# Keys times values in quarter tiles, and another order at the seam of two loops, in a three-stage sequence model kernel

## What is computed

```python
batch, n_heads, seq, head_dim = (4, 8, 768, 48)          # d_model = 384, d_ff = 1024
# 1. attention
for t in range(S):
    state = alpha[:, :, t, :, None] * state + np.einsum('bhd,bhe->bhde', k[:, :, t], v[:, :, t])
    y[:, :, t] = np.einsum('bhd,bhde->bhe', q[:, :, t], state)
# 2. x = y, heads side by side, [4, 768, 384]
theta = x @ w_theta
zr, zi = x * np.cos(theta), x * np.sin(theta)
u = x + np.einsum('ts,bsd->btd', w_tok_r, zr) + np.einsum('ts,bsd->btd', w_tok_i, zi)
x2 = u + np.maximum(u @ w_ch, 0.0)
# 3. h = relu(x2 @ w_in), halves u and v; v normed, mixed over tokens, plus bias; (u * v) @ w_out
```

## Time and profile before

| | us |
|---|---|
| median of three runs of the kernel before | 583.84 |
| the profiled execution | 583.59 |
| span of that execution, first to last instruction | 581.9 |
| TensorE busy in the span | 567.8 |
| VectorE busy | 395.5 |
| ScalarE busy | 247.3 |
| GpSimd busy | 225.9 |

### The profile page before, as it was taken

The page is one execution under the profiler, slowest core; times in us unless marked ns, Lnnn a source line. Parts: engine busy times, 40 slices in busy tenths (PEclk is TensorE's granted clock), DMA queues, the critical chain, the costliest instruction groups (busy, mean ns, idle before and its releaser), DMA issues.

```text
span 581.9 us, 13427 instructions
## 1 busy us (share of the span) xinstructions
PE 567.8 (98%) x5665; PEld 540.4 (93%) x5665; DVE 395.5 (68%) x627; ACT 247.3 (42%) x462; POOL 225.9 (39%) x184
## 2 busy tenths in 40 slices
PE   6899999999999999999999999999999999999997
PEld 5688899999999999999999989998999899989997
DVE  7988997787766766766644279977537752776253
ACT  2767565453544544544453135822432243134210
POOL 2465343342422522422513047363813471347131
PEclk9999999999999999999999999999999999999999
DMA  8953222322322332323033180200220022002002
GB/s 310 319 190 114 93 70 69 111 70 70 109 70 69 115 115 88 111 70 109 3 109 123 40 285 2 82 1 0 83 83 0 1 82 81 1 1 83 1 0 82
DMA packets 21228, 49.67 MB, mean 85 GB/s; under 512 B 1712, under 2 KB 16816, under 8 KB 20656
## 3 DMA queue, kind: packets, MB, share of 16 engines
q1 hardware_dynamic: 21168, 48.81, 24.3%
HBM read 39.37 MB, written 9.44 MB: 84 GB/s over the span
## 4 chain that ended last, share of the span: by engine, by line
PE 83%; DVE 9%; ACT 4%; issue 2%; POOL 2%; DMA 1%; SPq 0%; DVEq 0%; ACTq 0%
PE psY L525 20%; PE psC L557 6%; PE psC L481 5%; PE psY L700 4%; PE psY L651 4%; PE psY L661 3%; PE psS L429 3%; PE psF L641 3%; PE psS L700 3%; PE psF L700 3%; PE psY L641 2%; PE psS L651 2%; PE psS L661 2%; PE psF L661 2%; PE psF L455 2%
## 5 line engine op out<-in xcount | busy, mean ns | idle before, releaser
L1357 POOL TENSOR_TENSOR z_lo<-cos_sin,z_hi 128x768 fp32r<-128x768 f32 x23 | 43.9, 1907 | 88.6 <-ACT z_hi L814 88.6
L1431 POOL TENSOR_TENSOR gated_lo<-raw_gated,gated_hi 128x384 fp32r<-128x384 f32 x32 | 35.9, 1128 | 70.3 <-ACT gated_hi L956 69.2
L1344 POOL TENSOR_TENSOR akq<-akq 128x512 f32<-128x512 f32 x23 | 27.4, 1192 | 69.9 <-DVE akq L1023 69.9
L1364 POOL TENSOR_TENSOR u_lo<-u_f,u_hi 128x384 fp32r<-128x384 f32 x24 | 28.3, 1207 | 47.0 <-ACT u_hi L819 47.0
L525 PE MATMUL psY<-tok_r_hi,z_hi 128*128 128x384 f32 x123 | 43.2, 351 | 0.1
L525 PE MATMUL psY<-tok_i_hi,z_lo 128*128 128x384 f32 x123 | 41.2, 335 | 0.0
L525 PE MATMUL psY<-tok_i_lo,z_hi 128*128 128x384 f32 x123 | 41.2, 335 | 0.0
L525 PE MATMUL psY<-tok_i_hi,z_hi 128*128 128x384 f32 x123 | 41.2, 335 | 0.0
L525 PE MATMUL psY<-tok_r_hi,z_lo 128*128 128x384 f32 x123 | 41.1, 335 | 0.0
L525 PE MATMUL psY<-tok_r_lo,z_hi 128*128 128x384 f32 x123 | 41.1, 334 | 0.0
L956 ACT ACTIVATE gated_hi<-raw_gated 128x384 fp32r<-128x384 f32 x32 | 16.4, 526 | 57.9 <-DVE raw_gated L1266 57.3
(11 more groups left out here) (307 smaller groups left out, 1829.3 us busy)
## 6 DMA issues: line engine op xcount, KB each, us to landing
akq<-akq SPq DMA_DIRECT2D x22, 770.0 KB, 4.6
v<-v_in SPq DMA_DIRECT2D x24, 192.0 KB, 5.0
x_dram<-u_f SPq DMA_DIRECT2D x8, 576.0 KB, 3.7
out<-ot SPq DMA_DIRECT2D x24, 192.0 KB, 1.9
raw_x<-x_dram SPq DMA_DIRECT2D x3, 1152.0 KB, 5.1
raw_tok_r<-w_tok_rT SPq DMA_DIRECT2D x6, 384.0 KB, 7.0
raw_tok_i<-w_tok_iT SPq DMA_DIRECT2D x6, 384.0 KB, 8.1
raw_sp<-w_spT SPq DMA_DIRECT2D x4, 576.0 KB, 6.2
```

Source lines behind the costliest of these rows:

```text
L1357: pool.tensor_tensor(Z[c][1][:], trigs[g % 2][:], f(Z[c][0][:]), ALU.subtract).then_inc(z_lo, 1)
L1431: pool.tensor_tensor(GA[1][:, j, half(h)], ug[:, j, half(h)], f(GA[0][:, j, half(h)]), ALU.subtract).then_inc(g_lo, 1)
```

## The change

Four things. `keys_values` makes each pair's product in four quarters of 32 rows instead of two halves of 64: 16 matmuls a chunk instead of 8, for 20 chunks. In the slots of chunks 6 to 11 `scores` comes ahead of `turn_k`; as `turn_k` was what waited for the scaled keys, `scores` now waits for them itself. On ScalarE `tok_high(6)` and `tok_high(7)` move behind the sines of chunk 4, and `whole_turns(5)` and `copy_kT(6)` ahead of `keep_xT(5)`; at chunk 6 `copy_x(6)` comes ahead of `z_high(5)`. On VectorE, at chunk 5, `xT_low(5)` moves ahead of `decay_queries(6)`; at chunk 6 the order becomes `decays_back(7)`, `decay_queries(7)`, `xT_low(6)`, `scale_keys(7)`.

```diff
-TOKEN_HALVES = tuple(slice(32 * i, 32 * i + 32) for i in range(4))
+QUARTERS = tuple(slice(32 * i, 32 * i + 32) for i in range(4))
...
             def scores(g):
                 s = akq_of(g)[0]
+                pe.wait_ge(k_scaled, g + 1)
                 pe.wait_ge(q_scaled, g + 1)
...
                 for p in range(PAIRS):
-                    for h in range(2):
-                        rows = slice(64 * h, 64 * h + 64)
+                    for q, rows in enumerate(QUARTERS):
                         mm = pe.matmul(psK[rows, HD * p:HD * (p + 1)], kT[:, p, rows],
-                                       V[g % 2][:, HD * (2 * p + h):HD * (2 * p + h + 1)], start=True, stop=True)
+                                       V[g % 2][:, HD * (2 * p + q // 2):HD * (2 * p + q // 2 + 1)], start=True, stop=True)
...
                     if g < AHEAD:
+                        scores(g)
                         turn_k(g)
-                        scores(g)
...
                 if c:
                     whole_turns(c - 1)
-                if c == CHUNKS - 1:
-                    for i in SPLITS[c]:
-                        tok_high(i)
                 copy_x(c)
...
                 if 1 < c < CHUNKS - 1:
                     xT_high(c)
+                if c == CHUNKS - 1:
+                    for i in SPLITS[c]:
+                        tok_high(i)
                 if c > 1:
                     z_high(c - 1)
+                if c == CHUNKS - 1:
+                    whole_turns(c)
+                    copy_kT(c + 1)
                 keep_xT(c)
...
-                    if g < AHEAD:
+                    if g == CHUNKS:
+                        sines(g - 1)
+                        copy_x(g)
+                        z_high(g - 1)
+                    elif g < AHEAD:
                         whole_turns(g - 1)
                         copy_kT(g)
...
             def decay_queries(g):
+                dve.wait_ge(after_made, g + 1)
                 need(dve, decayed, g)
...
                     reduce_angle(c - 1)
                     scale_keys(c + 1)
+                    xT_low(c)
                     decay_queries(c + 1)
-                    xT_low(c)
                     multiply_z(c - 1)
...
                         multiply_z(g - 1)
-                        if g + 1 < AHEAD:
+                        if g == CHUNKS:
+                            decays_back(g + 1)
+                            decay_queries(g + 1)
+                            xT_low(g)
+                            scale_keys(g + 1)
+                        elif g + 1 < AHEAD:
                             decay_keys(g + 1)
                             decay_queries(g + 1)
                     if g + 1 < AHEAD:
                         make_x2(tile_of(b, c))
-                        xT_low(g)
+                        if g > CHUNKS:
+                            xT_low(g)
                         update_state(g)
```

More of the change, by code:

```diff
@@ L453, in attend @@
                         pr = slice(2 * HD * p, 2 * HD * (p + 1))
-                        for rows in TOKEN_HALVES:
+                        for rows in QUARTERS:
                             mm = pe.matmul(psO[rows, pr], Q[akq_of(g)[0]][:, p, rows], S[c % 2][:, p, :],
```

## The result

| | before | changed |
|---|---|---|
| median of 11 runs each, us | 584.00 | 586.64 |
| spread of the changed kernel's runs, us | | 584.78 to 587.81 |
| the profiled execution, us | 583.59 | 585.72 |
| its span, us | 581.9 | 584.0 |

The ratio is 1.0039 [1.0028, 1.0049]: the medians say 2.6 us slower, where 1.5 us faster was forecast. It lies outside the range, which ended at 584.3. One of the 11 runs of the kernel before took 799.13 us, and one of those made beside the experiments 1958.22; both are left out of the ratios. By this ratio the loss is 2.3 us.

A forecast was written before the change was run, and what follows sets the result against it. TensorE was taken as the bound, busy 567.8 of 581.9 us. Terms: +0.8 up to chunk 7, -0.50 at chunks 8 and 9, +0.23 at chunk 10, -2.0 behind, so -1.5: median 582.3, range 579.6 to 584.3.

The forecast's parts named there:

- Chunks 0 to 4 (5 sets) are paced by VectorE: nothing.: Chunks 0 to 4: VectorE sets the pace, so their five sets in quarters change the time by nothing.
- Part 1, 0.25 us a set: Keys times values in quarters: each set takes 0.35 to 0.39 us instead of 0.60, saving 0.25, bounds 0.21 and 0.30.
- The third rival: Quarters run at the halves' 37.5 ns a record, 0.60 us more per set: 593.0; slower 0.15, full price 0.02.
- Chunks 12 and 18: Their saved sets gain nothing: TensorE would only wait 0.25 us longer for z_lo at each.
- Part 2, 0.48 us at chunk 10: Scores before k's transposition: kT's later copy delays the low part of x, 0.23 us later instead of 0.25 earlier.
- Part 3, +0.8 us up to chunk 7: New order at chunks 5 and 6: VectorE and GpSimd alternate, so the angles of chunk 7 start 0.8 us late.
- The first rival: Chunk 5: GpSimd's scale_queries(6) gets through before VectorE's multiply_z(4), sum -3.0 us, 580.9; chance 0.25.
- A wait behind chunk 12 other than z_lo's: Sign of being wrong: behind chunk 12 only waits for z_lo were expected; no size given.
- The rule against small tiles: About 60 cycles per matmul whatever its width: 32 records would take about 0.8 us; weighed, but line 464's 12.3 ns decided.

The follow-up runs named there:

- after_loads_late: Changed kernel, quarters everywhere, with the loads of w_ch and the second half of the token weights issued behind those of v(4) and chunk 5's keys; 583.82 us.
- early_quarters: Kernel before with quarters in chunks 0 to 2 alone, old order everywhere; 586.08 us, ratio 1.0036.
- late_quarters: Kernel before with quarters from chunk 6 on only, old order everywhere; 581.04 us, ratio 0.9942.
- order_alone: Changed kernel with halves everywhere, so only the new order of instructions; 585.58 us, ratio 1.0022.
- late_quarters_scores_first: late_quarters with scores ahead of turn_k at chunks 6 to 11; 582.71 us, ratio 0.9979.
- tok_low_behind_mask: Changed kernel with halves in chunks 0 to 5 and VectorE's tok_low(6) and tok_low(7) moved behind the mask of chunk 6; 581.73 us.
- seam_turn_k_first: tok_low_behind_mask with turn_k ahead of scores again at chunks 6 to 11; 581.08 us, ratio 0.9951.
- after_late_quarters: Changed kernel with halves in chunks 0 to 5, quarters from chunk 6 on; 583.28 us, ratio 0.9988.
- chunk5_vector_order: Kernel before with quarters from chunk 6 on, ScalarE's new order, and VectorE's xT_low(5) ahead of decay_queries(6); 582.49 us, ratio 0.9977.

## Why the prediction was wrong, point by point

**"Chunks 0 to 4 (5 sets) are paced by VectorE: nothing."** This step failed. For matmul time it holds: in after_loads_late, with five early sets in quarters and no stop, the marks of chunks 1 to 4 are within 0.1 us of the kernel before. But an instruction also has to be fetched. I counted records only as time, and did not ask when they reach TensorE: 96 more of them ahead of 30 us, in a stretch whose DMA engines were full (the 0.91 of the earlier trace rows hinted at it), made TensorE run out for 2.4 us, and the clock fell to 0.82 and 0.76 behind it. Worth: 2.2 us at the mark of chunk 4 in the profiled run; 2.2 us between the medians of early_quarters and the kernel before; 2.8 us between those of the changed kernel and after_loads_late. The section Instruction fetch mechanics of the page "Runtime: NRT & Kernel Launch" of the Trainium skill describes a fetch in blocks of 16 KiB through a queue of the sequencer's own, and calls its cost "mostly hidden". The block size agrees with the packets seen; hidden it was in the kernel before and in after_loads_late, and in the changed kernel it was not, 2.4 us of it. The step of the prediction that failed, then, is this term: put at nothing, it measured 2.2 to 2.8 us.

**Part 1, 0.25 us a set.** Right. The timeline of the changed kernel at chunk 13:
```profile
163.53 0.55 PE L441 MATMUL psF<-v,kT 128*32 128x48 f32 x32
...
163.90 0.84 PE L455 MATMUL psF<-state,akq 128*32 128x96 f32 x32
```
32 records in 0.37 us, 11.6 ns each, instead of 16 in 0.60. The third rival is out. Chunks 14 to 16 and 19 to 22 each bring the marks 0.23 to 0.31 nearer, and late_quarters gains 2.8 us, where 12 counted sets would give 3.0. Chunks 12 and 18 gain nothing, as forecast, and TensorE's waits there for z_lo come to 0.5 us, against 0.1 in the kernel before; chain of work of the changed kernel at chunk 12 (start, us, what):
```profile
153.53 1.84 POOL z_lo L1371
...
155.42 3.39 PE psY L525 x18
```

**Part 2, 0.48 us at chunk 10 (0.23 later instead of 0.25 earlier).** Right at chunk 10 and incomplete. In order_alone, which saves no set there, chunk 10 costs 0.30 where the low part of x was forecast to cost 0.23, and in late_quarters_scores_first 0.55 where 0.48 was forecast. Missed was chunk 11, another 0.31 in order_alone, about half of which can be placed: in order_alone TensorE reaches line 465 0.85 us after line 456, instead of 0.68 in the kernel before, and VectorE's mask of that chunk ends only 0.15 us ahead of it. The rest of chunk 11 stays open. On the old seam the effect was 1.44 us, 0.56 of it at chunk 7. With the new order it was 0.8 us and nothing by chunk 7 (tok_low_behind_mask against seam_turn_k_first).

**Part 3, +0.8 us up to chunk 7.** Right in mechanism and, at full clock, in size. order_alone, profiled with its clock at 1.00, shows +0.75, by the very steps: `scale_queries(6)` 1.81 us long (forecast 1.85), z_lo(4) done at 64.06 (64.04), line 464 of chunk 6, there 465, at 67.81 (67.79) after a wait of 1.68 us, the second scan of chunk 6 held up to 72.99 (73.02). The first rival fell: VectorE went first. What was missed is the clock. In part of the runs it falls behind the wait for the mask, which gives 1.3 us more (after_late_quarters, above); the longer wait had been priced by its length alone. The median of order_alone lies 1.7 us above the kernel before, where its profiled run lost 1.3; that gap is not the clock's, for nine of its 12 runs had 0.999 or 1.000, and these spread over 584.8 to 585.8, as the runs of the kernel before spread over 1.0 us.

**A wait behind chunk 12 other than z_lo's.** I had named it as a sign of being wrong, and it came, in the changed kernel: the mark of chunk 13 is +3.91 after +3.09. Its timeline, with the lines in the order of cause:
```profile
158.45 1.23 DVE L1011 TENSOR_TENSOR_SCAN after<-akq,restart 128x516 f32<-128x516 f32 x1 [2.64 <-DMA akq<-akq]
...
160.77 4.33 POOL L1378 TENSOR_TENSOR u_lo<-u_f,u_hi 128x384 fp32r<-128x384 f32 x3 [5.40 <-ACT u_hi L819]
165.06 1.17 POOL L1358 TENSOR_TENSOR akq<-akq 128x512 f32<-128x512 f32 x1
...
166.34 1.16 PE L430 MATMUL psS<-akq 48*128 48x128 f32 x16 [0.92 <-issue]
```
The keys of a chunk landed late, so VectorE's scans met GpSimd's `u_lo`, `scale_queries` ended at 166.23 and TensorE started the scores at 166.34. The profile writes "issue", but the reader's input had only just come. In after_late_quarters, after_loads_late and order_alone chunk 13 shows no such step. The load was not issued late: SP issued it at 151.56 us in the changed kernel and at 151.51 in after_late_quarters. It took longer to land, as the DMA views of 145 to 160 us show (size, us to landing), changed kernel and after_late_quarters:
```profile
akq<-akq SPq DMA_DIRECT2D x1, 770.0 KB, 6.9
akq<-akq SPq DMA_DIRECT2D x1, 770.0 KB, 4.3
```
So the step comes from that load, and not from the order on the engines. Why that load took 6.9 us, and in how many of the 11 runs it did, is open.

**The sum by the marks** of the profiled run: +2.17 (fetch and clock up to chunk 4), +0.60 (seam), -0.30 (chunks 8 and 9), +0.62 (chunks 10 and 11), +0.82 (chunk 13 with its set), -0.73 (chunks 14 to 16), -1.07 (chunks 17 to 22): +2.11, the difference of the spans.

## What to carry to other kernels

An edit that adds instructions is to be checked where it costs no engine time as well: count the instructions ahead of each stretch in which the DMA engines are full, for the code comes through them too. A stall of TensorE is to be priced with the chance of a lower clock behind it, not by its length alone. And where VectorE and GpSimd exclude each other, a swap of two VectorE instructions can decide who goes first; chunk 5's swap alone cost 1.65 us in the trace and 2.1 in the median.

## What the runs showed of the hardware

- TensorE's code arrives in packets of 16 KB in a DMA queue of its own (45 packets before, 47 with 640 more records). Its fetch began at 30.31 us with the DMA engines at 1.06, and at 27.32 us once loads were moved. TensorE stopped for 2.1 to 2.4 us at its 961st record, and the row says only "<-issue".
- After stops of 2.1 and 2.4 us, and after 1.8 us of waiting in a stretch where TensorE was busy for 2.2 of 4 us, windows of 4 us showed a granted clock between 0.53 and 0.82, for 4 to 8 us in all. It is no certain consequence: chunk5_vector_order waited 2.28 us, with TensorE busy for 1.72 of 4, and kept 1.00. Runs of early_quarters at a mean clock of 0.994 took about 3 us more than those at 0.999 and 1.
- To the start of the next group, 32 fp32 records of 128x32 with 48 columns take 11.6 ns each, 16 records of 128x64 37.5 ns. The rule against small tiles that the prediction weighed (the section Instruction Overhead of "TensorEngine Tiling (Array Packing)" in the Trainium skill) does not hold for these.
- VectorE and GpSimd alternate once both have work with two SBUF inputs: 1.2 us becomes 1.8, 1.84 becomes 2.55. The rule of first come in the page "SBUF — State Buffer" of the Trainium skill, section Who interferes with whom, agrees with who led at the seam (VectorE at 60.70 against GpSimd at 60.86 in one kernel, GpSimd at 59.39 against VectorE at 59.68 in the other).
